# The last batch of an attention stage: which engine turns the first pair's weights, and where two output tiles stand

## The reference

```python
# stage 1, linear attention, per head (8 batches, 8 heads, 576 tokens, width 64)
q_s = softmax(q, over the width);  k_s = softmax(k, over the tokens)
x = q_s @ (k_s.T @ v)                      # heads side by side: (8, 576, 512)
# stage 2, MLP with a residual
y = x + relu(layernorm(x) * g_ln @ w_ch1) @ w_ch2      # 512 -> 2048 -> 512
# stage 3, four attention experts of width 64, the two best per token
for e in range(4):
    q, k, v = y @ wq[e], y @ wk[e], y @ wv[e]
    a = softmax(causal(q @ k.T / 8))
    out += gate[:, e] * (a @ v @ wo[e])
```

## Time and profile before

| what | value |
|---|---|
| three runs: median (lowest, highest) | 1236.82 us (1235.04, 1237.44) |
| the profiled execution, its time | 1237.43 us |
| the profiled execution, its span | 1235.6 us |
| TensorE busy | 1208.4 us, 98% of the span |
| VectorE, ScalarE, GpSimd busy | 54%, 31%, 18% |
| mean granted TensorE clock | 0.994 |
| last batch: its first scores begin | 1182.0 us |
| last product of TensorE ends | 1232.5 us |

### The profile page before, as it was taken

How to read it: one execution, slowest core, us unless ns; L and a number is a source line. 1 busy time by engine, 2 the same in 40 slices (tenths; PEclk the granted TensorE clock), 3 DMA queues, 4 the chain that set the end, 5 groups by cost and what they waited for, 6 DMA issues and landing times.

```text
span 1235.6 us, 19273 instructions
## 1 busy us (share of the span) xinstructions
PE 1208.4 (98%) x7064; PEld 1006.5 (81%) x7064; DVE 672.4 (54%) x1713; ACT 386.2 (31%) x871; POOL 218.3 (18%) x244
## 2 busy tenths in 40 slices
PE   8999999999999999999999999999998999999998
PEld 7877888888888888888888888888887888888875
DVE  5786365366365366356366332321357777776762
ACT  4462131131122121221222211112254554555554
POOL 2533000000000000000000000002136565456321
PEclk9999999999999999999999999999998999999999
DMA  8741460370280280270270130151057787887752
GB/s 184 184 107 39 117 101 5 97 121 5 73 145 5 73 146 2 76 141 6 77 132 13 40 76 27 35 117 37 16 148 218 193 245 207 247 241 200 189 158 78
DMA packets 346321, 133.45 MB, mean 108 GB/s; under 512 B 242545, under 2 KB 330609, under 8 KB 346225
## 3 DMA queue, kind: packets, MB, share of 16 engines
q1 hardware_dynamic: 345696, 132.18, 44.6%
q10 hardware_dynamic: 528, 0.00, 0.0%
HBM read 72.49 MB, written 42.86 MB: 93 GB/s over the span
## 4 chain that ended last, share of the span: by engine, by line
PE 86%; DVE 5%; SPq 3%; DMA 2%; ACT 2%; issue 1%; POOL 0%; DVEq 0%; ACTq 0%
PE hb L1523 31%; PE yb L1611 31%; PE sc L1523 13%; PE ob L1769 4%; PE pa L1540 3%; PE pa L1531 1%; SPq L719 1%; PE sc L1735 1%; DMA pt<-turned 1%; PE tb L1735 1%; ACT prob L1060 1%; DMA turned<-px 1%; SPq L571 1%; DMA vsb<-in_v_dram 1%; PE tb L1747 1%
## 5 line engine op out<-in xcount | busy, mean ns | idle before, releaser
L1314 DVE SCALAR_TENSOR_TENSOR hid_lo<-hb,hid_hi 128x512 fp32r<-128x512 f32 x144 | 99.5, 691 | 383.1 <-ACT hid_hi L942 383.1
L942 ACT ACTIVATE hid_hi<-hb 128x512 fp32r<-128x512 f32 x144 | 85.8, 597 | 614.8 <-PE hb L1523 614.8
L1611 PE MATMUL yb<-hid_hi,w_hi 128*128 128x512 f32 x576 | 226.5, 393 | 2.4 <-DVE hid_lo L1314 2.4
L1523 PE MATMUL hb<-xn_hi,w_hi 128*128 128x512 f32 (+1 forms) x580 | 228.1, 393 | 0.0
L1523 PE MATMUL hb<-xn_lo,w_hi 128*128 128x512 f32 (+1 forms) x580 | 225.1, 388 | 0.0
L1523 PE MATMUL hb<-xn_hi,w_lo 128*128 128x512 f32 (+1 forms) x580 | 225.0, 388 | 0.0
L1611 PE MATMUL yb<-hid_hi,w_lo 128*128 128x512 f32 x576 | 224.3, 389 | 0.0
L1611 PE MATMUL yb<-hid_lo,w_hi 128*128 128x512 f32 x576 | 224.1, 389 | 0.0
L1523 PEld LDWEIGHTS hb<-xn_hi,w_hi 128*128 128x128 f32 x580 | 108.8, 188 | 25.6 <-issue 2.2
L1611 PEld LDWEIGHTS yb<-hid_hi,w_hi 128*128 128x128 f32 x576 | 108.1, 188 | 25.0 <-issue 2.8
L1523 PEld LDWEIGHTS hb<-xn_hi,w_lo 128*128 128x128 f32 x580 | 108.9, 188 | 22.7
(11 more groups left out here) (219 smaller groups left out, 1811.3 us busy)
## 6 DMA issues: line engine op xcount, KB each, us to landing
qx<-in_q_dram SPq DMA_DIRECT2D x32, 288.0 KB, 5.4
ksb<-in_k_dram SPq DMA_DIRECT2D x8, 1024.0 KB, 5.7
vsb<-in_v_dram SPq DMA_DIRECT2D x32, 256.0 KB, 4.8
stage<-in_moe_w_ch_dram SPq DMA_DIRECT2D x16, 512.0 KB, 4.1
xn_lo<-ksb SPq DMA_DIRECT2D x128, 64.0 KB, 2.0
y_scratch<-ysb SPq DMA_DIRECT2D x32, 256.0 KB, 2.9
ysb<-xsb SPq DMA_DIRECT2D x128, 64.0 KB, 2.1
out_dram<-osb SPq DMA_DIRECT2D x32, 256.0 KB, 4.3
```

Source lines behind the costliest of these rows:

```text
L942: act.activation(HID[f % 2][0][:], hb[f % 2][:], ACT.Relu).then_inc(sems["hhi_a"], 1)
L1314: dve.scalar_tensor_tensor(out=lo[:], in0=hb[f % 2][:], scalar=0.0, in1=plain(hi[:]), op0=ALU.max, op1=ALU.subtract).then_inc(sems["hlo_v" ...
L1523: ins = pe.matmul(dst, l, r, start=(n == 0), stop=(n == len(terms) - 1))
L1611: ins = pe.matmul(yb[j][:], l, r, start=(f == 0 and m == 0 and not first), stop=(f == FT - 1 and m == 2), skip_group_check=True)
```

## The change

In the last batch the first pair (units n = 0 to 8) is no longer turned by TensorE, but as in the other batches: GpSimd writes PX, VectorE turns, SyncE writes and lands. The second pair is still turned by TensorE. The scores of the first pair (and of units 9 and 10) use TB in turn with SC[0:2], since TB is free of transposes until step 12; two score steps are formed at steps 0 and 4, as in other batches. The output tiles of the batch ahead move from steps 10 to 13 to steps 6, 7, 11 and 12. The sums (0, 0) move from step 9 to 10 and (0, 1) from step 12 to 15. The second pair's half 1 gets a PT of its own, PT_LAST, in the place of Y[0], which the last batch doesn't use.

```diff
+            PT_LAST = sb("pt_last", [P, 2 * CHUNK[1] // 32, NT, 32], F32, st)
...
+        FILL_LAST = {**{n: ("M", 4 + n) for n in range(4)}, 6: ("OUT", 0), 7: ("OUT", 1), 11: ("OUT", 2), 12: ("OUT", 3)}
...
-        WEIGH_LAST = {9: [(0, 0)], 12: [(0, 1)], 17: [(1, 1)], 21: [(1, 0)]}
+        WEIGH_LAST = {10: [(0, 0)], 15: [(0, 1)], 17: [(1, 1)], 21: [(1, 0)]}
...
-            f = (FILL_ODD if st[1] % 2 else FILL).get(n)
+            f = (FILL_LAST if last else FILL_ODD if st[1] % 2 else FILL).get(n)
...
+        def by_pe(k, shift, last):
+
+            return last and shift == 0 and TWOS[k][0] >= NS
...
-            return SC[:, 0:2, :] if turn or k % 2 == 0 else TB2
+            return SC[:, 0:2, :] if turn and n >= NS + 2 or k % 2 == 0 else TB2
...
-                        if not (last and shift == 0):
+                        if not by_pe(k, shift, last):
                             write_turned(st, shift, k)
 
                         j, of = (k - 1, shift) if k else (9, shift - 1)
-                        if (j, of) != (9, -1) if first else not (last and of == 0):
+                        if (j, of) != (9, -1) if first else not by_pe(j, of, last):
                             land(st, of, j)
...
-                    if last and lagging(n, T_LAG, True, last):
-                        u, _ = lagging(n, T_LAG, True, last)
+                    if last and NS <= n - T_LAG < UNITS:
+                        u = n - T_LAG
...
-                        if not (last and shift == 0):
+                        if not by_pe(k, shift, last):
                             turn_blocks(st, shift, k)
...
-                free = n if last else n - 2 + (n % NS == 0)
+                free = n if last and n >= NS + 4 else n - 2 + (n % NS == 0)
...
-                if turn:
-                    pe.wait_ge(pt_a, p * NS + ((NS, NS - SUBS[1][0])[h] if p else s1))
+                if turn and p:
+                    pe.wait_ge(pt_a, (NS, NS - SUBS[1][0])[h])
                 else:
                     for k in ((0, 1), (2, 3, 4))[h]:
                         nth = nth_turned(st, shift, 5 * p + k)
...
-                    if n < UNITS and unit(n, last)[1] % (2 if last else 4) == 0:
+                    four = not last or n < NS
+                    if n < UNITS and unit(n, last)[1] % (4 if four else 2) == 0:
                         scores(st, n, first, last)
-                        if not last and n % NS < NS - 1:
+                        if four and n % NS < NS - 1:
                             scores(st, n + 2, first, last)
-                    if last and lagging(n, T_LAG, True, last):
-                        transposes(st, lagging(n, T_LAG, True, last)[0])
+                    if last and NS <= n - T_LAG < UNITS:
+                        transposes(st, n - T_LAG)
...
-                            output(st, shift, x, bank(n), 4 if x == 0 else 0)
+                            output(st, shift, x, bank(n), {0: 3, 2: 4}.get(x, 0) if last else 4 if x == 0 else 0)
```

More of the change, by code:

```diff
@@ L134, in program @@
         y_in = sb("y_in", [P, KT, SP], F32, st2)
+        with ExitStack() as st:
+            PT_LAST = sb("pt_last", [P, 2 * CHUNK[1] // 32, NT, 32], F32, st)
         Y = [[sb(f"y{n}_{x}", [P, KT, SP], F32R, st2) for x in ("hi", "lo")] for n in range(2)]
@@ L299, in fill_at @@
                 return None if f and f[0] == ("V", CT) else f
-            f = (FILL_ODD if st[1] % 2 else FILL).get(n)
+            f = (FILL_LAST if last else FILL_ODD if st[1] % 2 else FILL).get(n)
             if f == ("V", CT) and st[1] % 2 == 0:
                 return None
-            if f is None or (f[0] == "OUT" and first) or (last and (f[0] == "V" or (f[0] == "M" and f[1] < 4))):
+            if f is None or (f[0] == "OUT" and first):
                 return None
@@ L425, in kept @@
             at = (s // 2 * 2 - SUBS[h][0]) * 4
-            to = PT[h][:, at : at + 4] if s == NS - 1 else PT[h][:, at + s % 2 : at + 8 : 2]
+            pt = PT_LAST if h else PT[h]
+            to = pt[:, at : at + 4] if s == NS - 1 else pt[:, at + s % 2 : at + 8 : 2]
             return to[:, :, 0 : TILES_OF[s], :].rearrange("p a j c -> p j a c")
@@ L859, in scale @@
             def scale(st, shift, k, last):
-                turn = last and shift == 0
+                turn = by_pe(k, shift, last)
                 if k == 0:
@@ L1070, in batch @@
                         output(st, 0, 0, out_bank_last(0), OUT_LAST)
-                    if last and lagging(n, T_LAG, True, last):
-                        u, _ = lagging(n, T_LAG, True, last)
+                    if last and NS <= n - T_LAG < UNITS:
+                        u = n - T_LAG
                         p, s = unit(u, last)
-                        act.wait_ge(p_t, u + 1)
-                        weighed_before(act, st, 0, p, s)
+                        act.wait_ge(p_t, u - NS + 1)
+                        if half_of(s) == 0:
+                            weighed_before(act, st, 0, p, s)
                         act.copy(kept(u, last), kept_from(u, last)).then_inc(pt_a, 1)
@@ L1450, in masked @@
                 if last and n >= NS:
-                    dve.wait_ge(p_t, s + 1)
+                    need2(dve, "pscale_g", st, 0, s + 1)
                 elif lagging(n, NS, first, False):
@@ L1742, in transposes @@
                 need2(pe, "pscale_g", st, 0, u + 1)
-                far = 1 if s == NS - 1 or (u and unit(u - 1, True)[1] == NS - 1) else 2
-                if u >= far:
-                    pe.wait_ge(pt_a, u - far + 1)
+                far = 1 if s == NS - 1 or unit(u - 1, True)[1] == NS - 1 else 2
+                if u - NS >= far:
+                    pe.wait_ge(pt_a, u - NS - far + 1)
                 for j in range(TILES_OF[s]):
@@ L1763, in weighted @@
                     need2(pe, "otlo_v", st, shift - 1, nth + 3)
+                pt = PT_LAST if turn and p and h else PT[h]
                 v, tiles = V[(st[1] + shift) % 3], TILES_OF[s1 - 1]
@@ L1769, in weighted @@
                         ins = pe.matmul(OB[nth % 2][e * HD : (e + 1) * HD, at : CHUNK[h]].rearrange("p (a c) -> p a c", c=32), v[:, j, (2 * p + e) * HD : (2 * p + e + 1) * HD],
-                                        PT[h][:, at // 16 + e :: 2, j, :], start=(j == 0), stop=(j == tiles - 1), skip_group_check=True)
+                                        pt[:, at // 16 + e :: 2, j, :], start=(j == 0), stop=(j == tiles - 1), skip_group_check=True)
                 ins.then_inc(sems["o_mm"], 1)
```

## The result

Over 20 runs each the changed kernel has a median of 1241.62 us against 1236.78 us: a ratio of 1.0041, 95% interval 1.003 to 1.0051. In a second set of runs, 1240.76 against 1236.29 us, it was 1.0049 (1.0031 to 1.0067). So by the medians it is 4.5 to 4.8 us slower, more than the 0.2% that I had named, and above the range of 1235.2 to 1240.8 us. The forecast of +1.5 us, within 0.2%, was wrong.

The account below looks back on a forecast made before the run. The last batch was taken as bound by TensorE's own work, with some waiting and slow clock. Later sums and tail gave +0.85 us, half clock +0.6: +1.5 us, 1238.3 us on the median, range 1235.2 to 1240.8.

Parts of the forecast that it names:

- What is removed: Last batch: 25 first-pair transposes go, 3.7 us of TensorE, with nine ScalarE copies and the scores' mask waits around 1192 us.
- half clock at 1195 us: Slow-clock stretch from 1195.0 to 1198.5 us before the change, some 1.5 us, expected to go.
- To the sums (0, 0): Last batch: TensorE idles 3.5 us for the landing of k = 1; sums begin at 1203.6, 1.8 us later than before.
- To the sums (0, 1): Last batch: second wait of 3.6 us, for the landing of k = 4; sums begin at 1215.5 instead of 1208.06 us.
- From there to the end: Sums (0, 1) and unit 16's scores end at 1218.3 us; all behind is as before, so the sum is +0.85 us.
- The clock: Half clock again after both waits: 0.6 us after the first; 1.5 us after the second counted as taken over, not added.
- the 1217.44 us of unit 13: Start of unit 13's transposes before the change, compared with 1218.3 us after it for the +0.85 us.
- The clock decides: Rival: half clock on all of sums (0, 0), (0, 1) and again on (1, 1), +3.5 us: 1240.3 us; chance 0.20.
- Slow landings: Rival: both first-pair landings take the median 4.2 us, writes 0.5 us more: 1240.5 us; chance 0.07.

Follow-up runs that it names:

- kept clock: Changed kernel plus 13 unused products of 128x512 ahead of each of the two waits for landings: 1238.32 us, ratio 1.0023.
- (0, 0) at 11: Changed kernel with sums (0, 0) moved to step 11 and sums (0, 1) to step 17: ratio 1.0004.
- (0, 0) at 12: Changed kernel with sums (0, 0) moved to step 12 and (0, 1) to 17, SyncE's order kept: ratio 0.9997.
- the two versions made from it: Sums at steps 12 and 17 plus unused products ahead of units 13 and 14's transposes: 1234.51 us; also OUT 2's store behind k = 4's landing: 1235.31 us.

## Why the prediction was wrong, point by point

- **What is removed.** Right: x25 transposes instead of x50, and no half clock at 1195 us in any profile of after.
- **To the sums (0, 0).** Right, though put 0.3 to 0.7 us too late: 20.9 to 21.3 us into the batch, forecast 21.6. The order on SyncE that I named sets it; the landing of k = 1 took 3.0 us where I had put 3.3.
- **To the sums (0, 1).** The mechanism was right, the size off: forecast 33.5 us into the batch, 34.1 with the 0.6 us of slow clock, measured 34.4 to 35.1. The term that was mis-sized is `land` of k = 4: 3.4 us put, 4.8 to 4.95 us measured (1.5 us). I had argued that the queue carries little else; the change itself puts a 512 KB landing and a store ahead of it. Another term hides a part of this: the last write was there 2.1 us behind its issue, where I had put 2.8.
- **From there to the end.** Right: forecast 17.9 us from the start of (0, 1) to the end of the last product, measured 17.9 to 18.4 us.
- **The clock.** Right after the two waits: half clock in four profiles of four. The second step that failed, beside the landing of k = 4, is the other side of this balance, as I put it: "against this stands the same 1.5 us on sums (1, 1) before, which I count as taken over, not added". It was not there to be taken over in every execution, and neither was the half clock at 1195 us, which stands in the 1217.44 us of unit 13 that I reckoned from: (0, 1) began at 26.0 us in the first profile and at 24.4 or 24.5 in the other three. The first profile of before is the slowest of four (53.6 against 50.4, 50.6 and 52.2 us). With a mean of 51.7 us, 1.9 us less than I reckoned from, the sum is +1.5 (forecast) + 1.9 (the starting point) + 1.5 (the landing) - 0.5 (sums (0, 0) earlier than forecast) = +4.4 us, the difference of the means; the terms not named here (writes 0.7 us quicker, tail and clock after (0, 0) some 0.5 us slower) nearly cancel. Shown by the four profiles of either kernel: the same short waits in the kernel before sometimes come with half clock and sometimes don't, and the waits of 3.5 to 4.1 us of the changed kernel always did. Not shown: the share. By the medians, as estimated above, the starting point was 1.3 us too long and the last batch after is 2.0 us over the forecast 55.1 us.
- **The rivals.** "The clock decides", 1240.3 us at 0.20, had the right side, and its condition, (0, 1) and (1, 1) both at half clock, was not what was met: in the changed kernel (1, 1) ran at full clock (2.23 us). What lay behind the 4.8 us was a slower landing and a kernel before that is usually quicker than its first profile. "Slow landings", 1240.5 at 0.07, was right for one landing of two: that of k = 4 took more than its 4.2 us, that of k = 1 only 3.0.
- **Open.** Why the four writes of k = 2 took 3.1 to 3.2 us to issue in five profiles (kept clock, (0, 0) at 11, (0, 0) at 12, and the two versions made from it) and 1.8 us in the changed kernel's, though SyncE's instructions up to there are the same.

## What to carry to other kernels

Before reckoning a change from a profile, ask which of its costs come and go between executions: one profile of a kernel with short idle stretches may show a half clock that its median doesn't have, so take a second and a third profile of the kernel before first. When work moves from the bound engine to a way through other engines and DRAM, place what consumes it by the arrival time and not by the step count of a steady stage: one entry in a table of steps, (0, 1) at 17 instead of 15, was worth 3.7 us here. And on an in-order DMA queue a landing that waits for its own writes holds up everything behind it; let another step's issues stand between them.

## What the runs showed of the hardware

- Granted clock: with TensorE waits of 3.5 to 4.1 us the clock fell to half in every profile of the changed kernel, within the wait or up to 1.0 us behind its end; the two short groups of waits in the kernel before (1.25 and 1.84 us of idle time) were followed by half clock in two, none, none and one case of two, from one execution to the next, with the same instructions.
- Unused products in the waits kept the granted clock at its full level in all four kernels that had them in their last batches, and the changed kernel's time fell by 2.4 us with them.
- The landing of k = 4, 320 KB, took 4.2 to 4.95 us in the ten profiles in which a store or a 512 KB landing was issued within 2 us ahead of it, and 3.1 to 3.6 us in the four others that have it. That of k = 9, as large and with neither near it, took 2.8 to 2.9 us in the changed kernel.
